# One TensorE product of 256 columns beside each of 16 gate chunks, with two waits moved, one warming product less and the weight loads in halves

## What is computed

```python
# attention: B, H, S, D = 4, 8, 768, 48
for t in range(S):
    y[:, :, t] = q[:, :, t] @ state
    state = state + beta[t] * outer(k_n[t], v[t] - state.T @ k_n[t])
# network: 3072 tokens, 384 -> 2048 -> 384
h = x @ w_in
g = where(h > 0, h, exp(min(h, 0)) - 1)
x2 = g @ w_out
# experts: 8, top 2, 384 -> 1024 -> 384
logits = x2 @ w_gate + log1p(exp(x2 @ w_noise)) * noise
out[token] += weight * (maximum(x2 @ w1[e], 0) @ w2[e])
```

## Time and profile before

| | |
|---|---|
| runs | 1159.55, 1160.15, 1161.24 us, median 1160.15 |
| profiled execution | 1161.79 us, span of the instructions 1159.8 us |
| PE busy / PEld busy | 1118.3 us (96%) / 1072.3 us (92%) |
| DVE / ACT / POOL busy | 641.7 / 471.9 / 365.1 us |

### The profile page before, as it was taken

How to read it: one execution, slowest core, us unless ns; L and a number is a source line. 1 busy time by engine, 2 the same in 40 slices (tenths; PEclk the granted TensorE clock), 3 DMA queues, 4 the chain that set the end, 5 groups by cost and what they waited for, 6 DMA issues and landing times.

```text
span 1159.8 us, 28066 instructions
## 1 busy us (share of the span) xinstructions
PE 1118.3 (96%) x11054; PEld 1072.3 (92%) x11054; DVE 641.7 (55%) x1552; ACT 471.9 (41%) x1068; POOL 365.1 (31%) x386
## 2 busy tenths in 40 slices
PE   6799999999999999999999999999999999999996
PEld 5687787878999999999999999999999999999995
DVE  7968778753464656565564657523434343434432
ACT  5336666873333333334334344323333333333331
POOL 6888993550002102020202102322323232222233
PEclk9999999999999999999999999999999999999998
DMA  8455666557995111010101012472424243434221
GB/s 173 125 135 123 171 159 147 150 138 269 379 354 170 41 42 42 20 42 20 42 20 42 34 32 89 168 231 85 156 88 156 92 148 103 139 102 137 62 68 53
DMA packets 83015, 137.63 MB, mean 119 GB/s; under 512 B 11082, under 2 KB 70450, under 8 KB 81882
## 3 DMA queue, kind: packets, MB, share of 16 engines
q1 hardware_dynamic: 68906, 88.37, 26.6%
q0 software_dynamic: 12992, 28.75, 7.8%
q10 hardware_dynamic: 1008, 18.97, 4.3%
HBM read 82.35 MB, written 53.77 MB: 117 GB/s over the span
## 4 chain that ended last, share of the span: by engine, by line
PE 75%; DVE 1%; issue 0%; ACT 0%; POOL 0%; ACTq 0%; POOLq 0%
PE ps_x L1493 18%; PE ps_x L1583 18%; PE ps_h L1482 18%; PE ps_h L1561 17%; PE ps_r L1541 2%; PE ps_r L1532 2%; DVE hg L1901 0%; ACT hg L1691 0%; POOL out_dram L1448 0%; DVE w_parts L1864 0%; PE ps_r L1600 0%; DVE x_raw L1894 0%; PE ps_r L1510 0%; ACT yT_d L1709 0%; PE ps_r L1508 0%
## 5 line engine op out<-in xcount | busy, mean ns | idle before, releaser
L1583 PE MATMUL ps_x<-hg,w_parts 128*128 128x400 f32 x1152 | 230.2, 346 | 0.0
L1493 PE MATMUL ps_x<-w_parts,hg 128*128 128x400 f32 x1152 | 229.6, 345 | 0.0
L1482 PE MATMUL ps_h<-xg,w_parts 128*128 128x384 f32 x1152 | 222.3, 338 | 0.0
L1561 PE MATMUL ps_h<-xg,w_parts 128*128 128x400 f32 x1116 | 220.6, 345 | 1.1 <-DVE w_parts L1864 1.1
L1493 PEld LDWEIGHTS ps_x<-w_parts,hg 128*128 128x128 f32 x1152 | 209.6, 188 | 0.0
L1901 DVE SCALAR_TENSOR_TENSOR hg<-ps_h,hg 128x400 fp32r<-128x400 f32 x128 | 73.6, 575 | 243.1 <-ACT hg L1691 240.2
L1482 PEld LDWEIGHTS ps_h<-xg,w_parts 128*128 128x128 f32 x1152 | 204.0, 188 | 2.5 <-DVE elu_parts L1758 2.5
L1561 PEld LDWEIGHTS ps_h<-xg,w_parts 128*128 128x128 f32 x1116 | 202.6, 188 | 4.0 <-issue 3.1
L1583 PEld LDWEIGHTS ps_x<-hg,w_parts 128*128 128x128 f32 x1152 | 206.0, 188 | 0.0
L1428 POOL DMA_INDIRECT xs_scratch<-x,rows_now x48 | 49.6, 1033 | 393.8 <-DVE rows_now L1838 293.8
L1691 ACT ACTIVATE hg<-ps_h 128x400 fp32r<-128x400 f32 x128 | 64.7, 505 | 254.7 <-PE ps_h L1561 252.8
(11 more groups left out here) (179 smaller groups left out, 1325.7 us busy)
## 6 DMA issues: line engine op xcount, KB each, us to landing
xs_scratch<-pads SPq DMA_DIRECT2D x2, 5502.0 KB, 42.7
x_rows<-xs_scratch SPq DMA_DIRECT2D x17, 614.1 KB
kqT<-in_kqT_dram SPq DMA_DIRECT2D x48, 192.0 KB, 4.1
carried<-in_w_dram ACTq DMA_DIRECT2D x3, 3072.0 KB
w_raw<-in_w_dram ACTq DMA_DIRECT2D x3, 3072.0 KB
xs_scratch<-pads SPq DMA_DIRECT2D x6, 1375.5 KB, 17.0
out_dram<-pads SPq DMA_DIRECT2D x1, 4800.0 KB, 30.1
xs_scratch<-pads SPq DMA_DIRECT2D x6, 786.0 KB
```

Source lines behind the costliest of these rows:

```text
L1482: mm = nc.tensor.matmul(ps_h[f % 2][:, 0:TB], wi[:, 1 - a, k, f * P:(f + 1) * P], xr[:, b, k, :], start=(i == 0), stop=(i == len(passes) - 1))
L1493: mm = nc.tensor.matmul(ps_x[t][:, 0:DG], act_r[:, f % RING, a, t * P:(t + 1) * P], wo[:, b, f, :], start=(f == 0 and i == 0), stop=(f == ...
L1561: mm = nc.tensor.matmul(ps_h[f % 2][:, 0:TR], w1, xg[:, b, k, :], start=(m == 0), stop=(m == len(passes) - 1))
L1583: mm = nc.tensor.matmul(ps_y[k][:, 0:TR], w2r[i][:, a, s, k * P:(k + 1) * P], hg[:, s % RING, b, :], start=(s == 0 and m == 0), stop=(s == ...
```

## The change

Five edits, all in `attention_outputs`:

- PE does `keep_clock(256, 7, 256)` after each of the 16 `turn_output_weights(f)`. It writes columns 256 to 511 of PSUM bank 7, behind the 256 columns of the gate's sums.
- `KEEP_BUSY` is 27 instead of 26, so five products of 192 columns stand before the loop instead of six.
- PE's wait for `gate_taken` moves from the front of these products to the first product of keys of chunk 2, inside the loop; ACT's `take_gate` moves behind six `place`.
- On ACT, the copies of turned chunks 0 and 1 stand before the second square root instead of behind it.
- Weight pieces 0 to 5 are loaded in two halves of 512 columns, one half in each of a pair's two steps; ACT waits for both.

```diff
-KEEP_BUSY = 26
+KEEP_BUSY = 27
...
-            def load_weights(i):
+            def load_weights(i, h=0):
...
-                    given = w_io[:, at:W_CUTS[i + 1]]
+                    half_way = (W_CUTS[i + 1] - at) // 2
+                    at += h * half_way
+                    to, given = to[:, h * half_way:(h + 1) * half_way], w_io[:, at:at + half_way]
...
-                    for i in pieces[n % 2:n % 2 + 1]:
-                        load_weights(i)
+                    if len(pieces) == 1 and pieces[0] < W_EARLY:
+                        load_weights(pieces[0], n % 2)
+                    else:
+                        for i in pieces[n % 2:n % 2 + 1]:
+                            load_weights(i)
...
-            def keep_clock(columns):
+            def keep_clock(columns, bank=0, at=0):
...
-                nc.tensor.matmul(psum[:, 0, 0:columns], masks[:, 0, 0], masks[:].rearrange("p g s t -> p (g s t)")[:, 0:columns],
+                nc.tensor.matmul(psum[:, bank, at:at + columns], masks[:, 0, 0], masks[:].rearrange("p g s t -> p (g s t)")[:, 0:columns],
...
                     turn_output_weights(f)
+                    keep_clock(256, 7, FT1 * GATES)
                     if f:
                         gate_columns(f - 1)
...
                 else:
+                    if n == 2 and c == 0:
+                        pe.wait_ge(gate_taken, 1)
 
                     pe.wait_ge(masked, (2 * n + c) * 2)
...
             gate_columns(FT1 - 1)
-            pe.wait_ge(gate_taken, 1)
             for j in range(KEEP_BUSY, BLK):
...
-                act.wait_ge(w_loaded[i], 16)
+                act.wait_ge(w_loaded[i], 32 if i < W_EARLY else 16)
...
+                for f in chunks_with(i):
+                    take_turned(f)
                 if i == WIDE_BLOCKS - 1:
                     root_of(1)
-                for f in chunks_with(i):
-                    take_turned(f)
-            take_gate()
             act.wait_ge(cleared, len(by_pool))
...
             for r in (1, 3):
                 place(0, r)
+            take_gate()
             take_solved(0, 0)
```

## The result

The changed kernel takes 1166.08 us, the median of nine runs (1161.63 to 1171.65), beside 1161.24 us for the kernel before in the same nine rounds (1158.89 to 1165.12). The ratio is 1.0039, 95% interval 1.0023 to 1.0055: about 4.5 us slower. It is inside the forecast range and of the forecast sign, but half the forecast 8.9 us.

The account below looks back on a forecast made before the run. PE's row of gate chunks and warming products was taken to bound the first solve. Terms -2.65 + 12.75 - 0.47 - 0.69 = +8.9 us on the median 1160.15 gave 1169.1 us; range 1152 to 1172.

Parts of the forecast that it names:

- What bounds the kernel: Before the loop, PE's own row of gate chunks and warming products holds the first solve, from about 36.5 us on.
- The clock before 80 us: Everything before about 80 us runs at the lower level, 1.2 GHz, whatever the clock column says; the rest at 2.4.
- root: Copies of chunks 0 and 1 before ACT's second root: chunk 1 turned at about 33.85 instead of 36.5, 2.65 us gained.
- products: On PE's row, 15 of the 16 added products cost 0.85 us each: 12.75 us (9.75 to 13.8).
- wait and warming row: Before the loop: 0.47 us gained by not waiting for the gate's copy, 0.69 by one warming product less.
- stalls: PE's 1.34 us stall inside block 9 may be hidden by slower work ahead of it; counted 0, bound -1.3.
- slow products: Leading case: added products stay at the lower clock level on PE's row; 1169 us, chance 0.66.
- halves: SP's six more transfers are hidden behind its waits, and PE doesn't wait for POOL: nothing, 0 to -1 us.
- early rise: Rival: the added products lift the clock among the gate chunks, near chunk 3; 1152 us; clock up early, chance 0.23.
- up before the tenth chunk: Clock rise among the gate chunks: zero effect at n near 9.6 slow chunks; earlier is faster, 1152 to 1159 us.
- that price: With a rise near chunk 3, twelve chunks give back 5.4 us and three blocks some 2 us.
- Kept busy without a break: Skill's rule: continuously busy TensorE gets the full clock, so denser chunks should lift it; the prediction said the trace disagrees.

Follow-up runs that it names:

- two products then one: Changed kernel with two added products beside each of chunks 0 to 7 and one beside each of 8 to 15; 1161.78 us, ratio 0.9979 to the kernel before.

## Why the prediction was right, and where it was off

**What bounds the kernel.** Right. PE's row of chunks and warming products held the first solve, and what moved the solve moved the end: behind the loop nothing changed. The loop itself isn't as constant as the prediction had it: over the 14 traces it took 188.92 to 193.83 us.

**The clock before 80 us.** Right for what the trace showed: the column of 1.00 was no measurement there, and durations of like records dated the level. The products at the lower level took 0.85 us each, to the hundredth.

**The sum.** In the profiled run, from chunk 0 to the solve, +6.24 us instead of +8.9. Its terms are: root -2.88 (forecast -2.65), products +12.8 (+12.75), wait and warming row -1.50 (-1.16), stalls -2.20 (0). The term that failed is the stall in block 9, counted at 0 with a bound of -1.3: with slow products ahead of it, it was gone, and so was its neighbour of 0.36 us in block 10. Block 9 took 1.48 us instead of 3.03 and block 10 took 1.48 instead of 2.13. The warming row shrank by 0.85 us instead of 0.69, but the same six products took 5.06, 4.26 and 4.21 us in three traces, so that much differs from trace to trace. One by one over many runs, the terms are: products 10.6 us (forecast 12.75), root -1.9 (-2.65), wait and warming product -0.8 (-1.16), not told from nothing, and halves -2.2 (0). Multiplied, 1.0091 x 0.9984 x 0.9993 x 0.9981 = 1.0049, beside the measured 1.0039 and 1.0034; the difference is smaller than the intervals. So the halves are the second term that was mis-sized. Of the reasons given for nothing, SP's 56.2 us of waits spoke only against a loss. The other, that PE doesn't wait for POOL, isn't refuted; by what way the halves help stays open.

**The rivals.** The step that failed is "here each 0.85 us is followed by 1.8 us of transposes and 16-column products of the kind that never did it". One product beside a chunk does lift the clock, in part of the runs: 14 of 22 had a mean clock that shows an early rise taken back. I had treated slow products and an early rise as two cases of which one would come true, each with a chance. They are two kinds of run of the same program, and the median lies between them. This is the smaller part of why 4.5 us were measured and not 8.9: the median of all 22 runs, 1166.3 us, is 1.7 us under that of the eight without such a sign, while 2.7 us were already missing in the profiled run, which kept the lower level. With the spread inside each kind the 1.7 us aren't secured. The bound that I worked out, up before the tenth chunk, fits the one trace with an early second rise: about six chunks were slow (0, 1 and 5 to 8), and the run took 1158.20 us, 4.1 under the kernel before, where the formula gives 4.8. One term of that price was too large: a block takes 1.22 us at the upper level and 1.48 at the lower one, so three give 0.8 us and not 2.

**Kept busy without a break.** The prediction weighed a rule of the Trainium skill, "TensorE: Matmul & The Clock Gate", section on why this matters for your kernels: TensorE kept busy without a break gets the full clock. The profiled run disagrees. PE is busy for 5.00 us of each 5 from 35 to 85 in its windows, and its added records still took 634 ns each:

```profile
L540 PE MATMUL psum<-masks 128*128 128x256 f32 x32 | 17.0, 634 | 0.0
```

In the trace of two products then one the column itself shows it: PE is busy for 5.00 us of each 5 from 50 to 85, and the granted clock is 0.50 in every one of these windows. So by these traces busy time alone doesn't tell the level. Nor do two products beside each chunk: at the lower level behind the stall they had it back within one chunk in one trace and not within three in two others. Whether transposes count is not shown.

**What the change was worth.** The two kernels with two products beside each chunk are about 6 us faster than the kernel before; in three of their 18 runs the mean clock (0.990, 0.984 and 0.971) shows the level taken back for longer. Without any product it is 4.6 us, and the intervals overlap.

## What to carry to other kernels

Where the clock column of a profile starts at full, check it against durations of the same instruction early and late; a product that is meant to warm the engine costs double until it works (here 0.85 us at the lower level and 0.42 at the upper one), so one such product a chunk was worse than none, and two were better than one and not told apart from none. When a kernel's outcome depends on whether the clock rises, give the cases as shares of its runs, and look at the mean clock run by run before believing one trace.

## What the runs showed that I had not expected

- Twice the filler was faster: in the same rounds 1156.78 us with 32 products, 1166.84 with 16, and 1157.86 with none.
- PE's stall behind small products (1.34 us before, rows 5) was there, with 0.8 to 1.9 us, wherever chunks ran fast or had no filler, and was absent where slow products stood ahead of it. Its cause is open.
- Five traces show an early rise. At the stall the level fell in four of them and stayed in one, and three of the four had the same instructions up to there as the one that stayed.
- Chunk 0 was turned at 32.1 to 35.2 us in the 14 traces, in a stretch that no edit touches. Single traces can't be compared to better than that at their start.
